# A three-stage fp32 kernel on one core: logits over 104 columns, and other places for the steps between MLP and experts

## What is computed

```python
attn_out = _attn_ref(**attn_kwargs)                     # (2, 8, 768, 40): gated linear attention
x = attn_out.transpose(0, 2, 1, 3).reshape(1536, 320)

h = x @ w_in                                            # MLP: 320 -> 2048
x = np.maximum(0.01 * h, h) @ w_out                     # 2048 -> 320

logits = x @ w_gate                                     # 8 experts, all of them used for every token
P = np.exp(logits - logits.max())
for _ in range(8):                                      # Sinkhorn rounds
    P /= P.sum(1, keepdims=True) + 1e-09
    P /= P.sum(0, keepdims=True) + 1e-09
    P *= N / E
for e in range(E):
    out += P[:, e:e + 1] * (np.maximum(x @ w1[e], 0.0) @ w2[e])
```

## Time and profile before

| | us |
|---|---|
| median of three runs | 961.64 (961.07 to 963.73) |
| the profiled execution | 964.44 |
| its span, first to last instruction | 962.7 |
| PE busy | 941.3 (98%) |
| DVE busy | 654.5 (68%) |
| POOL busy | 403.4 (42%) |
| ACT busy | 365.7 (38%) |

### The profile page before, as it was taken

How to read it: one execution, slowest core, us unless ns; L and a number is a source line. 1 busy time by engine, 2 the same in 40 slices (tenths; PEclk the granted TensorE clock), 3 DMA queues, 4 the chain that set the end, 5 groups by cost and what they waited for, 6 DMA issues and landing times.

```text
span 962.7 us, 16689 instructions
## 1 busy us (share of the span) xinstructions
PE 941.3 (98%) x6519; PEld 896.6 (93%) x6529; DVE 654.5 (68%) x1090; ACT 365.7 (38%) x662; POOL 403.4 (42%) x473
## 2 busy tenths in 40 slices
PE   8999999999979899999999999999999999999998
PEld 5899888888769899999999999999999999999998
DVE  7677665457758899976666666666676667666664
ACT  5675443344444433233432333333233234233221
POOL 4364141045072545475651754384165347436000
PEclk9899999999989999999999999999999999999999
DMA  7961222001011101111211120121112102110000
GB/s 146 198 110 21 61 61 66 1 21 46 0 34 33 34 14 54 34 32 36 61 39 34 34 66 1 34 66 34 34 33 67 33 2 66 34 34 1 29 29 28
DMA packets 82796, 42.39 MB, mean 44 GB/s; under 512 B 54270, under 2 KB 82302, under 8 KB 82718
## 3 DMA queue, kind: packets, MB, share of 16 engines
q1 hardware_dynamic: 82510, 41.23, 16.6%
q10 hardware_dynamic: 208, 0.11, 0.0%
HBM read 39.13 MB, written 2.11 MB: 43 GB/s over the span
## 4 chain that ended last, share of the span: by engine, by line
PE 86%; DVE 7%; ACT 3%; issue 2%; DMA 1%; SPq 1%; DVEq 0%; ACTq 0%
PE psB L1650 11%; PE psB L1652 11%; PE psB L1651 11%; PE psA L1633 8%; PE psA L1636 8%; PE psA L1634 8%; PE psA L1635 8%; PE psA L1565 7%; PE psB L1584 2%; PE psB L1586 2%; PE psB L1585 2%; PE psA L1463 2%; PE psB L1484 2%; DVE leaky L1194 1%; PE psB L1591 1%
## 5 line engine op out<-in xcount | busy, mean ns | idle before, releaser
L670 POOL TENSOR_TENSOR wst<-raw_w,wst 128x128 fp32r<-128x128 f32 (+2 forms) x192 | 161.2, 852 | 324.7 <-ACT wst L858 172.5
L1650 PE MATMUL psB<-w2s,gh 128*128 128x320 f32 x768 | 238.5, 311 | 0.0
L1651 PE MATMUL psB<-w2s,gh 128*128 128x320 f32 x768 | 237.3, 309 | 0.0
L1652 PE MATMUL psB<-w2s,gl 128*128 128x320 f32 x768 | 237.3, 309 | 0.0
L975 ACT ACTIVATE gh<-part 128x512 fp32r<-128x512 f32 x192 | 111.0, 626 | 315.7 <-DVE part L1378 310.9
L1633 PE MATMUL psA<-xop,wst 128*128 128x256 f32 x672 | 191.3, 285 | 7.2 <-DVE pg L1315 5.7
L1384 DVE SCALAR_TENSOR_TENSOR gl<-part,gh 128x512 fp32r<-128x512 f32 x192 | 153.7, 841 | 63.0 <-ACT gh L975 62.7
L1634 PE MATMUL psA<-xop,wst 128*128 128x256 f32 x672 | 191.1, 284 | 0.0
L1635 PE MATMUL psA<-xop,wst 128*128 128x256 f32 x672 | 191.0, 284 | 0.0
L1636 PE MATMUL psA<-xop,wst 96*128 96x256 f32 x672 | 190.9, 284 | 0.0
L1650 PEld LDWEIGHTS psB<-w2s,gh 128*128 128x128 f32 x768 | 144.6, 188 | 0.2 <-issue 0.2
(11 more groups left out here) (196 smaller groups left out, 1386.7 us busy)
## 6 DMA issues: line engine op xcount, KB each, us to landing
raw_w<-in_moe_w_dram SPq DMA_DIRECT2D x32, 320.0 KB, 3.2
raw_w<-in_moe_w_dram SPq DMA_DIRECT2D x32, 256.0 KB, 2.6
raw_w<-in_moe_w_dram SPq DMA_DIRECT2D x96, 64.0 KB, 2.5
qs<-in_q_dram SPq DMA_DIRECT2D x12, 160.0 KB, 3.0
ks<-in_k_dram SPq DMA_DIRECT2D x12, 160.0 KB, 3.4
vz<-in_v_dram SPq DMA_DIRECT2D x12, 160.0 KB, 3.6
og<-in_o_gate_dram SPq DMA_DIRECT2D x12, 160.0 KB, 3.8
out_dram<-acc SPq DMA_DIRECT2D x5, 320.0 KB, 2.2
```

Of the source, the lines that this page charges most:

```text
L670: return pool.tensor_tensor(dst, raw, high.bitcast(F32), ALU.subtract)
L1650: pe.matmul(bank, gh[:, slot, cols], w2[:, f, 0, :], start=first, stop=False)
L1651: pe.matmul(bank, gh[:, slot, cols], w2[:, f, 1, :], start=False, stop=False)
L1652: last = pe.matmul(bank, gl[:, slot, cols], w2[:, f, 0, :], start=False, stop=end)
```

## The change

It does the following.

- wgf, the gate weights, becomes 104 columns wide (LW = 13 * E). POOL fills columns 8 to 103 with zeros at the start (pad_ok). Each logits matmul runs over 104 columns; each next one overwrites the zeros that the one before left in its place.
- The early logits are taken to pg in group f = 6 of the last MLP block, ahead of x2_rest_low(1), not at the end of DVE's MLP queue. PE waits for this (lg_max 1) before p34 of pair 0, no longer before the first product.
- x2_kept goes from ACT to POOL, where rest_high(tb) makes both copies, in the place of second_high(tb). ACT's counts per block become 6, POOL's 2.
- ACT's x2_high(tb - 1) goes to f = 7 of the same block (was f = 0 of the next), and for tb = 1 out of pair 0; x2_high_sums(1) goes into middle(0). DVE's x2_rest_low goes to f = 6 (was 7), x2_low_direct to f = 7 (was f = 0 of the next block), x2_low_sums(0) to f = 0. In pair 0 DVE makes x2_low_sums(1) ahead of the three read_y.
- x2_first(2) goes to middle(3), ahead of high_of(3, .); it was behind it, ahead of the greatest logit.
- In every pair PE makes p26 before p1. column_sums, the late logits and the matmuls of the greatest logit stand behind behind(n, 1), no longer before behind(n, 0). norm_columns stands behind the two low_of.
- PE's waits in front of p1 are shorter: pair 4 waits for max_ok, not p_exp; two pairs behind a round it waits until the column sums are read (sink + 5), not for the whole round (+ 8).

```diff
@@ -68,6 +68,7 @@
     HT = TB // 2
     NPROD = 7
     PREP = [0, 2, 1, 3]
+    LW = 13 * E
     BP = NTB * PP
     NP = E * BP
     ROUND_AT = [5, 6, 7, 9, 10, 11, 13, 14]
@@ -93,7 +94,7 @@
 
 
         ident = sb("ident", [P, P], F32)
-        wgf = sb("wgf", [P, KT + 1, E], F32)
+        wgf = sb("wgf", [P, KT + 1, LW], F32)
         pg = sb("pg", [P, NT, E], F32)
         rs = sb("rs", [P, NT], F32)
         all_ones = sb("all_ones", [P, P], F32)
@@ -208,8 +209,7 @@
 
         h_ps = psA
         y_ps = psB
-        early_ps = psA[:, HB + 1, 0:(NTB - 1) * JT * E].rearrange("p (t e) -> p t e", e=E)
-        late_ps = psA[:, 0, HT:HT + JT * E].rearrange("p (t e) -> p t e", e=E)
+        early_ps, late_ps = psA[:, HB + 1, :], psA[:, 0, HT:]
         col_ps = psA[:, 0, HT:HT + NT * E]
         top_ps = psA[0:1, 0, HT:HT + P]
         max_ps = psA[:, 0, HT:HT + 1]
@@ -285,6 +285,7 @@
         spare_ok = sem("spare_ok")
         pool_step = sem("pool_step")
         wg_in = sem("wg_in")
+        pad_ok = sem("pad_ok")
         h_ready = sem("h_ready")
         hs_ok = sem("hs_ok")
         leaky_ok = sem("leaky_ok")
@@ -296,7 +297,7 @@
         xd = sem("xd")
         xa = sem("xa")
         xp = sem("xp")
-        XD, XA = 15, 7
+        XD, XA, XP = 15, 6, 2
         x2_ready = sem("x2_ready")
         lg_ready = sem("lg_ready")
         lg_max = sem("lg_max")
@@ -314,7 +315,7 @@
         g2 = sem("g2")
         o_used = sem("o_used")
         sink = sem("sink")
-        ROWS_NORMED, SINK_STEPS = 4, 8
+        ROWS_NORMED, COLUMNS_READ, SINK_STEPS = 4, 5, 8
         col_sums = sem("col_sums")
         acc_scaled = sem("acc_scaled")
         o_ready = sem("o_ready")
@@ -544,10 +545,10 @@
                     if n == U_IT + 3:
                         first_w1(KT)
             for a in range(KT):
-                sp.dma_start(wgf[:, a, :], w_gate[a * HK:a * HK + P, :]).then_inc(wg_in, 16)
+                sp.dma_start(wgf[:, a, 0:E], w_gate[a * HK:a * HK + P, :]).then_inc(wg_in, 16)
                 for side in range(2):
                     rows = slice(side * DR + a * R32, side * DR + (a + 1) * R32)
-                    sp.dma_start(wgf[rows, KT, :], w_gate[a * HK + P:(a + 1) * HK, :]).then_inc(wg_in, 16)
+                    sp.dma_start(wgf[rows, KT, 0:E], w_gate[a * HK + P:(a + 1) * HK, :]).then_inc(wg_in, 16)
             sp.wait_ge(xlo_done, NU)
             for p in PREP:
                 load_mlp_pair(p)
@@ -577,6 +578,7 @@
                 pool.affine_select(out=tile[:], in_=tile[:], compare_op=keep_if, fill=fill, base=base,
                                    pattern=[[step, tile.shape[1]]], channel_multiplier=rows).then_inc(consts, 1)
 
+            pool.memset(wgf[:, :, E:], 0.0).then_inc(pad_ok, 1)
             pool.wait_ge(consts, 2)
             where(head_rows, ALU.is_ge, 0.0, 0, -PARTS)
             where(at_row, ALU.not_equal, 1.0, -M0, -1)
@@ -698,11 +700,13 @@
                 low_of(two(w[mid, 1, 3:, :]), two(raw[mid, 1, :, :]), two(w[mid, 1, 3:, :])).then_inc(pair_ready, 1)
                 pool.wait_ge(pair_ready, r + 1)
 
-            def second_high(tb):
+            def rest_high(tb):
 
                 pool.wait_ge(xd, XD * tb + 8)
+                pool.tensor_copy(xop_of(tb, 0)[2 * R32:3 * R32], xraw_of(tb, 2)[2 * R32:3 * R32]).then_inc(xp, 1)
+                pool.wait_ge(xp, XP * tb + 1)
                 pool.tensor_copy(xop_of(tb, 2)[R32:2 * R32], xraw_of(tb, 2)[2 * R32:3 * R32]).then_inc(xp, 1)
-                pool.wait_ge(xp, tb + 1)
+                pool.wait_ge(xp, XP * (tb + 1))
 
             def scale_acc(tb):
 
@@ -715,11 +719,11 @@
                 mlp_low(p)
             pair_low(HALVES, 0)
             pair_low(HALVES, 2)
-            second_high(0)
-            second_high(1)
+            rest_high(0)
+            rest_high(1)
             pair_low(HALVES, 1)
             pair_low(HALVES, 3)
-            second_high(2)
+            rest_high(2)
             for p in PREP:
                 pair_low(HALVES + 1, p)
             pool.wait_ge(sink, SINK_STEPS * ROUNDS)
@@ -877,18 +881,10 @@
                 act.wait_ge(y_read, (KT + 1) * (NTB + tb + 2))
                 act.copy(xraw_of(tb, 2)[DR:P, 4:6, :], ysum[0:DR, tb, 0, :].rearrange("p (n t) -> p n t", t=HT)).then_inc(xa, 1)
 
-            def x2_rest_high(tb, dst):
+            def x2_first(tb):
 
                 act.wait_ge(xd, XD * tb + 8)
-                act.copy(dst, xraw_of(tb, 2)[2 * R32:3 * R32]).then_inc(xa, 1)
-
-            def x2_kept(tb):
-
-                x2_rest_high(tb, xop_of(tb, 0)[2 * R32:3 * R32])
-
-            def x2_first(tb):
-
-                x2_rest_high(tb, xop_of(tb, 2)[0:R32])
+                act.copy(xop_of(tb, 2)[0:R32], xraw_of(tb, 2)[2 * R32:3 * R32]).then_inc(xa, 1)
 
             def x2_high(tb):
 
@@ -932,12 +928,10 @@
                         if tb > 0 and f == 3:
                             x2_low_side(tb - 1)
                         if tb > 0 and f == 5:
-                            x2_kept(tb - 1)
-                        if tb > 0 and f == 6:
                             x2_first(tb - 1)
+                        if tb > 0 and f == 7:
+                            x2_high(tb - 1)
                         if tb > 1 and f == 0:
-                            x2_high(tb - 2)
-                        if tb > 1 and f == 1:
                             x2_high_sums(tb - 2)
 
 
@@ -997,9 +991,9 @@
                 if s + 1 < STAGES and at == 11:
                     pair_w2_high(s + 1, 1)
                 if n == 0:
-                    x2_high(1)
+                    x2_high_sums(1)
                 if n == 3:
-                    x2_kept(2)
+                    x2_first(2)
                 if n == 4:
                     x2_high(2)
 
@@ -1017,12 +1011,9 @@
                     pair_s_high(s + 1, n // 2 - 2)
                 if s + 1 < STAGES and at == 11:
                     pair_s_high(s + 1, 1)
-                if n == 0:
-                    x2_high_sums(1)
                 if n == 1:
                     x2_low_side(2)
                 if n == 3:
-                    x2_first(2)
                     act.wait_ge(max_ready, 1)
                     act.activation(gmax[:, 1:2], max_ps, ACT.Copy, scale=-1.0).then_inc(max_ok, 1)
                     act.wait_ge(max_ok, 1)
@@ -1253,25 +1244,29 @@
             def x2_rest_low(tb):
 
                 rest, kept = xop_of(tb, 2)[2 * R32:3 * R32], xop_of(tb, 0)[2 * R32:3 * R32]
-                dve.wait_ge(xa, XA * tb + 3)
-                dve.wait_ge(xp, tb + 1)
+                dve.wait_ge(xa, XA * tb + 2)
+                dve.wait_ge(xp, XP * (tb + 1))
                 dve.tensor_tensor(rest, xraw_of(tb, 2)[2 * R32:3 * R32], kept.bitcast(F32), ALU.subtract).then_inc(xd, 1)
 
             def x2_low_direct(tb):
 
                 high, low, y = xop_of(tb, 0).bitcast(F32), xop_of(tb, 1), ysum[:, tb, 1:, :]
-                dve.wait_ge(xa, XA * tb + 5)
+                dve.wait_ge(xa, XA * tb + 4)
                 dve.tensor_tensor(low[:, 0, :], y[:, 0, 0:HT], high[:, 0, :], ALU.subtract).then_inc(xd, 1)
                 dve.tensor_tensor(low[:, 2:4, :], halves_of(y[:, 1, :]), high[:, 2:4, :], ALU.subtract).then_inc(xd, 1)
 
             def x2_low_sums(tb):
 
                 high, low, raw = xop_of(tb, 0).bitcast(F32), xop_of(tb, 1), xraw_of(tb, 1)
-                dve.wait_ge(xa, XA * tb + 7)
+                dve.wait_ge(xa, XA * tb + 6)
                 dve.tensor_tensor(low[:, 4:, :], raw[:, 4:, :], high[:, 4:, :], ALU.subtract).then_inc(xd, 1)
                 dve.tensor_tensor(low[:, 1, :], raw[:, 1, :], high[:, 1, :], ALU.subtract).then_inc(xd, 1)
                 dve.wait_ge(xd, XD * (tb + 1))
                 dve.sem_inc(x2_ready, 1)
+
+            def logits_in(bank, tiles):
+
+                return bank[:, 0:tiles * E].rearrange("p (t e) -> p t e", e=E)
 
             def mlp_block(half, tb, done=0):
 
@@ -1294,11 +1289,14 @@
                             x2_rest_sums(tb - 1)
                         if f == 5:
                             x2_main_two(tb - 1)
+                        if f == 6 and tb == NTB - 1:
+                            dve.wait_ge(lg_ready, 1)
+                            dve.tensor_copy(pg[:, 0:(NTB - 1) * JT, :], logits_in(early_ps, (NTB - 1) * JT)).then_inc(lg_max, 1)
+                        if f == 6:
+                            x2_rest_low(tb - 1)
                         if f == 7:
-                            x2_rest_low(tb - 1)
+                            x2_low_direct(tb - 1)
                         if tb > 1 and f == 0:
-                            x2_low_direct(tb - 2)
-                        if tb > 1 and f == 1:
                             x2_low_sums(tb - 2)
 
             leak(0, 0)
@@ -1311,8 +1309,6 @@
             mlp_block(0, 2)
             for tb in range(NTB):
                 mlp_block(1, tb)
-            dve.wait_ge(lg_ready, 1)
```

(36 more changed lines are left out.)

## The result

The changed kernel takes 965.9 us (median of 7 runs, 965.44 to 967.85), the kernel before 962.22 beside it (7 runs, 961.07 to 964.07). The ratio is 1.0043, 95% interval 1.0029 to 1.0057: slower by 3.7 us by the medians and by 4.1 by the ratio. That is inside the range on record, 956.5 to 967 us, and outside the forecast's own, 960 to 964.5. The profiled executions are 965.9 (span 964.2) after and 964.44 (span 962.7) before, 1.5 us apart.

A forecast was written before the change was run, and what follows sets the result against it. DVE's queue was taken as the bound from the MLP's end to the last round; -0.6 - 5.3 + 2.0 + 0.2 + 0.6 + 3.9 + 0.2 + 0.1 = +1.1 gave 962.7 us, own range 960 to 964.5, whole range 956.5 to 967.

The forecast's parts named there:

- rival 2: Before read_y, each of nine DVE meetings costs a whole POOL instruction: contention 6.0, wait near 8, 966.8 us; chance 0.28.
- The rounds: In the round pairs, norm_columns behind low_of leaves DVE's 0.7 us wait open eight times: +3.9, bounds +0.5 and +5.8.
- Contention: Ahead of read_y, DVE's steps meet POOL at the shared port: 3.0 us, bounds 0 and 6; +0.2 against before.
- The wait in front of behind(1, 0), with its clock: PE waits there 4.7 us until read_y ends, plus 0.6 for half clock, of 0 to 1.7.
- The base: Behind the logits, the median run has no half clock, so its 1.7 us are gained only against the profiled one.
- The ysum wait: Up to the end of pair 0, ysum is read earlier and PE's wait of 0.6 goes: -0.6.
- the term's +2.0: In group 7, DVE's x2_low_direct(1) newly waits for ACT's x2_high(1): +2.0 us.
- 104 columns: In the logits, streaming 104 columns costs 0 to 0.2 us for a block, 0.1 taken for all.
- (1): From the MLP's end through the rounds, DVE isn't behind; contention falls on steps with room: 955.7 us; chance 0.26.
- (3): Behind the logits, 104 columns do not hold the clock: 1.7 us in one block of three, median 962.7; within forecast's 0.44.
- (4): Beyond the rounds DVE's delay goes on, 0.14 us in each of 80 pairs, 11 us; chance 0.02.
- POOL's zeroing: At the kernel's start, the zeros put 0.2 us on the path, bounds 0 and 0.4.

The follow-up runs named there:

- e1: The changed kernel with norm_columns put back ahead of the two low_of, nothing else undone: 959.57 us, ratio 0.9981 to the kernel before.
- e7: The changed kernel with the copy of the kept rows made by ACT again in group 5, not POOL: 967.59 us, ratio 1.0057 to the kernel before.
- e5: The kernel before with only the gate weights padded and zeroed by POOL, and logits streamed over 104 columns: 960.25 us, ratio 0.9985.
- e4: The changed kernel with POOL held back from pair_low of pair 3 until ysum is read: 963.19 us, ratio 1.0025 to the kernel before.
- e11: The kernel before with only the early logits' copy moved into group 6 of the last MLP block, ahead of x2_rest_low: 958.20 us, ratio 0.9960.

## Where the prediction was right and where it was wrong, point by point

It gave 962.7 us and slower by 1.1; it is slower by 3.7. The 965.9 lies inside the range of 956.5 to 967, which reached so far for rival 2's sake (966.8), and outside the forecast's own 960 to 964.5. By the 0.3% that it named as the least it can tell, the outcome is "slower", to which it gave 0.30, and not "same", 0.44. That the range held is in part luck, since rival 2's conditions came true only in part (below). The mechanism was right: DVE's queue is the bound, norm_columns behind low_of is what turns a gain into a loss (e1 against after: 6.0 us), and the waits came where they were expected. Four terms were off.

**The rounds: +3.9 expected, +6.7 measured.** The wait was sized well: PE idles 3.65 us more. What the term lacked is the clock in these pairs, though not all of it is added: e7, with full clock there, is only 2.0 us shorter. I gave the wait in front of behind(1, 0) a term for it and those in front of p1 none, though one came out at 1.9 us and the expectation named a wait of about 2. Two of them (1.67 and 1.88 us) were followed by 3.41 us at 0.50 each, and PE was busy 3.02 us longer. Waits of 1.52 in the earlier trace rows, 1.2 in e1 and 1.0 in most kernels were followed by none, and neither were those of 1.67 and 1.91 in e7: a wait of this length can bring half clock and need not. The stretch from the first to the last column sums took 71.8 us (333.1 to 404.9) where the earlier trace rows have 65.1 and I expected 68 to 70. The waiting itself isn't spread over eight pairs as the sum had it: DVE idles about 0.7 in front of low_of in every one of them, but PE meets it in three.

**Contention: 3.0 expected ahead of read_y, about 4.7 measured.** Each step less its shortest of all runs: x2_low_direct 0.96 and 1.10, low_of 0.79, x2_low_sums 0.53 and 1.34 (1.47 and 1.75, for 0.94 and 0.41). The bounds of 0 and 6 held it. x2_rest_low went the other way, 2.31 for the 3.37 of before. From the start of x2_rest_low to the end of read_y DVE took 19.7 us (270.05 to 289.79) for the 18.3 of the working, and it began at 272.5 on the clock of before, not 270.9. Hence read_y ended at 292.3 on that clock, 3.1 after the 289.2 of the text.

**The wait in front of behind(1, 0), with its clock: 4.7 + 0.6 expected, 6.25 + 2.0 measured.** It is within the 3 to 7 given. PE got there 1.6 later than worked out, at 286.1 for 284.5, of which 0.87 is a wait for pair 0's first addition that isn't in the sum: DVE had to wait 1.71 us for ACT and then do two slowed steps before it. Pair 0 itself was reached at 272.5 on the clock of before, for the 272.3 expected.

**The base: "the median has no such stretch".** I took from three runs and one profile that the half clock behind the logits is not in the median. e5 says otherwise: padding alone is worth 1.5 us in the median of 12 runs, and the mean clock of its runs is the higher. Counted in, the sum would have been about -0.4, and further from the result; this error hid a part of the others.

Against the profiled execution the same working gave -4.5 up to pair 7 (measured -2.85) and +3.9 behind it (+6.7): off by 1.65 and 2.8, together 4.4 us.

**A slip.** Its waits and half clock add up to 14.25 us (9.7 and 4.55), not to some 13.8; nothing else was worked out from that.

**What held.** The ysum wait fell, 0.4 for 0.6. DVE waits for ACT ahead of x2_low_direct, 1.71 us for the term's +2.0. DVE's wait of 0.70 ahead of low_of is there in round pairs. 104 columns take no more time than 8: the block starts at 223.50 and what follows at 226.10, and before it was 225.99 and 228.58.

**The rivals.** (1), that DVE is not behind, is out: the waits of PE between 290 and 405 us sum to 5.2 (1.03, 1.67, 0.59, 1.88), over the 3 that was its mark. (2), the port in full, gave 966.8 and is nearest to 965.9, but for a part only: its contention of 6 and its wait near 8 came out at 4.7 and 6.25 (just over its own mark of 6), and without the clock of the rounds it would have missed too. That such steps are slowed, e4 shows directly. (3) is out: the granted clock is 1.00 behind the first two blocks in after and in all ten experiments that have 104 columns. (4) is out: from the start of pair 16 PE is busy for 554.08 us in both kernels, and it is 557.5 us to the end of the span in after, 557.3 before.

**Not settled.** That POOL's zeroing costs 0.2 at the start was not measured by itself; e5 with it is faster. Whether p26 first is worth anything in these kernels stays open too, at 1.3 us inside the intervals.

## What to carry to other kernels

When a second engine's queue is full, ask of each step moved in it which idle time it filled where it stood: norm_columns cost nothing while it stood in the 0.7 us in which DVE waits for ACT, and 6 us when it stood behind it. A wait taken from the engine that seems to be the bound pays only as far as that queue gets shorter (3.8 of 8.5 us in e11), so move out of it what nobody needs yet, and have its supplier do its part first: three moves of whole steps and one wait of POOL turned +0.4% into -1.0%. And every wait that a sum leaves on TensorE needs its own term for the clock: here 0 or 1.7 us for a wait of 1.7 to 1.9, of which a part is taken back where PE would have waited for the other queue anyway (e7).
